# Attention and feed-forward in one kernel: feed-forward work per step as a constant, or as a fixed step length less the step's attention work

## The reference

```python
scores = scale * np.matmul(q, k.transpose(0, 1, 3, 2))
kth = np.partition(scores, -32, axis=-1)[..., -32:-31]
scores = np.where(scores >= kth, scores, -1e9)
attn = softmax(scores)                      # with 1e-9 added to the sum
x = (attn @ v) as (2304, 512)
h = x @ w_in;   x = np.maximum(0.01 * h, h) @ w_out      # layer 0, 512 -> 2048 -> 512
h = x @ w_in2;  g = where(h >= 1, h, where(h <= -1, 0, (h + 1) ** 2 / 4))
out = g @ w_out2                                         # layer 1
```

## Time and profile before

| | |
|---|---|
| median of 3 runs | 1160.88 us (1160.45 to 1161.57) |
| the profiled execution | 1158.78 us |
| its span, first to last instruction | 1156.8 us |
| TensorE (PE) busy | 1092.0 us, 94% |
| VectorE (DVE) busy | 872.2 us, 75% |
| ScalarE (ACT) busy | 792.0 us, 68% |
| GpSimd (POOL) busy | 472.1 us, 41% |
| chain that ended last, by engine | PE 79%, DVE 8%, ACT 6%, POOL 2%, issue 2%, DMA 2% |

### The profile page before, as it was taken

How to read it: one execution, slowest core, us unless ns; L and a number is a source line. 1 busy time by engine, 2 the same in 40 slices (tenths; PEclk the granted TensorE clock), 3 DMA queues, 4 the chain that set the end, 5 groups by cost and what they waited for, 6 DMA issues and landing times.

```text
span 1156.8 us, 21227 instructions
## 1 busy us (share of the span) xinstructions
PE 1092.0 (94%) x7568; PEld 1003.4 (87%) x7568; DVE 872.2 (75%) x1914; ACT 792.0 (68%) x1827; POOL 472.1 (41%) x500
## 2 busy tenths in 40 slices
PE   5557998899999999999999999999999999999998
PEld 3336888799989999999998879998899999999998
DVE  7999978889899998999979979988994005300234
ACT  7887989877798777887779758678786224322332
POOL 5645559652363332642236324134441234222322
PEclk9969999999999999999999989999999999999999
DMA  7998998788667788788666656656456677787774
GB/s 246 348 344 297 378 323 293 272 307 302 217 218 256 246 309 294 284 293 289 236 227 243 242 186 241 209 194 208 151 193 227 202 253 255 254 292 254 254 248 135
DMA packets 90680, 295.51 MB, mean 255 GB/s; under 512 B 10065, under 2 KB 13777, under 8 KB 90577
## 3 DMA queue, kind: packets, MB, share of 16 engines
q1 hardware_dynamic: 86544, 289.45, 71.2%
q10 hardware_dynamic: 4032, 4.72, 1.1%
HBM read 255.85 MB, written 38.27 MB: 254 GB/s over the span
## 4 chain that ended last, share of the span: by engine, by line
PE 79%; DVE 8%; ACT 6%; POOL 2%; issue 2%; DMA 2%; SPq 0%; POOLq 0%; ACTq 0%; DVEq 0%
PE ps_f L936 21%; PE ps_f L944 20%; PE ps_f L937 20%; PE ps_av L895 7%; DVE top L1223 4%; DVE work L1227 3%; PE ps_s L856 3%; PE ps_t L872 2%; PE ps_t L878 2%; PE ps_t L856 1%; DMA raw<-wd 1%; DVE part_r L1250 1%; ACT probs L1064 1%; POOL gate L747 1%; ACT scores L1035 1%
## 5 line engine op out<-in xcount | busy, mean ns | idle before, releaser
L1223 DVE MAX8 top<-work 128x8 f32<-128x576 f32 x432 | 310.6, 744 | 0.2
L936 PE MATMUL ps_f<-xy,w_ring 128*128 128x384 f32 (+2 forms) x896 | 288.8, 322 | 4.0 <-ACT part_o L1119 2.0
L936 PE MATMUL ps_f<-gate,w_ring 128*128 128x384 f32 (+2 forms) x896 | 286.7, 320 | 0.0
L944 PE MATMUL ps_f<-gate,w_ring 128*128 128x384 f32 (+2 forms) x896 | 281.7, 314 | 3.4 <-POOL gate L747 3.3
L944 PE MATMUL ps_f<-xy,w_ring 128*128 128x384 f32 (+2 forms) x896 | 280.8, 313 | 1.3 <-POOL xy L757 0.6
L937 PE MATMUL ps_f<-gate,w_ring 128*128 128x384 f32 (+2 forms) x896 | 281.0, 314 | 0.0
L937 PE MATMUL ps_f<-xy,w_ring 128*128 128x384 f32 (+2 forms) x896 | 280.2, 313 | 0.0
L1227 DVE MATCH_REPLACE8 work<-top,work 128x576 f32<-128x576 f32 x288 | 213.5, 741 | 0.0
L747 POOL TENSOR_TENSOR gate<-part_r,gate 128x384 fp32r<-128x384 f32 (+2 forms) x112 | 101.4, 906 | 240.0 <-ACT gate L1123 239.5
L936 PEld LDWEIGHTS ps_f<-xy,w_ring 128*128 128x128 f32 x896 | 169.2, 189 | 17.1 <-issue 9.6
L1258 DVE TENSOR_TENSOR y_acc<-ps_f,y_acc 128x384 f32<-128x384 f32 (+2 forms) x56 | 27.7, 495 | 199.1 <-PE ps_f L944 199.0
(11 more groups left out here) (85 smaller groups left out, 1846.2 us busy)
## 6 DMA issues: line engine op xcount, KB each, us to landing
w_ring<-w_split SPq DMA_DIRECT2D x408, 512.0 KB, 4.2
w_split<-w_ring SPq DMA_DIRECT2D x40, 512.0 KB, 6.1
raw<-wd SPq DMA_DIRECT2D x64, 256.0 KB, 5.4
w_split<-xy SPq DMA_DIRECT2D x24, 512.0 KB, 4.8
v_sb<-vd SPq DMA_DIRECT2D x32, 320.0 KB, 5.9
kq<-kqd SPq DMA_DIRECT2D x16, 480.0 KB, 3.7
kq<-kqd SPq DMA_DIRECT2D x15, 416.0 KB, 5.7
out_t<-y_acc ACTq DMA_DIRECT2D x12, 192.0 KB, 4.1
```

Of the source, the lines that this page charges most:

```text
L936: pe.matmul(out, w[:, 0, m], high, start=first, stop=False)
L944: mm = pe.matmul(out, w[:, 0, m], low, start=False, stop=end)
L1223: op = dve.max(top[:, t % TOP_SLOTS, 8 * r:8 * r + 8], source(t, r))
```

## The change

The constant FILL is taken out. Each of the steps 41 to 151 now adds STEP_NS less `attention_ns(s)`, a sum of fixed prices for the scores, the transposition and the values that the step holds. Earlier steps add FIRST_FILL as before. Nothing else of the program is edited; what else differs follows from the plan.

```diff
-FILL = 4275.0
+STEP_NS = 5950.0
...
+def attention_ns(s):
+
+    scores = sum(score_step(it) == s for it in ITEMS)
+    moved = [2 * KC + 1 if not it.mixed else KC + 2 for it in ITEMS if out_step(it) == s]
+    widths = [GROUP_WIDTH[gp // PAIRS % 2] for gp in range(GROUPS) if values_step(gp) == s]
+    return 1160.0 * scores + sum(109.0 * n + 100.0 for n in moved) + sum(20 * w / 2.4 + 300.0 for w in widths)
...
-        credit += FILL if s >= READY[1] else FIRST_FILL
+        credit += STEP_NS - attention_ns(s) if s >= READY[1] else FIRST_FILL
```

## The result

| | before | after |
|---|---|---|
| median | 1160.68 us (4 runs beside those of after) | 1169.53 us (4 runs, 1168.70 to 1170.11) |
| ratio to before | | 1.0078 [1.0062, 1.0094] |
| profiled execution, span | 1158.78, 1156.8 us | 1169.38, 1167.6 us |
| steps 41 to 151 | 677.42 us | 680.90 us |
| the tail | 253.45 us | 259.85 us |

The change makes the kernel 0.8% slower: 8.9 us, where 4.4 us less were forecast. The first view is the page of the kernel after, its busy time and its chain by engine.

A forecast was written before the change was run, and what follows sets the result against it. TensorE was taken to bound the kernel. Its losses in steps 41 to 151 were to fall from 13.7 to 5.9 + 2.0 + 1.0 + 0.4 = 9.3 us, so 1160.88 - 4.4 = 1156.5 us, range 1152.5 to 1162.5.

The forecast's parts named there:

- What bounds the kernel, and the views: TensorE bounds steps 41 to 151 and the tail; the change can only move time lost between its items.
- Point 1: Steps 41 to 151: TensorE's step lengths become more even, standard deviation 1.22 us instead of 1.64.
- Point 2: Three hidden units, 6.24 us, leave steps 41 to 151 and enter the tail: net 0.
- Point 3: Five places where score and transposition follow each other with little or no cover: 5.9 us lost together.
- Point 4: Output unit 3b1o0 opens in step 115 and waits for gates: 2.0 us lost instead of 2.87, clock kept.
- Point 5: Other late copies and gates, laid to VectorE lags over 33 us, mostly go: 1.0 us kept, bounds 0 and 5.
- Point 6: Weight loads on SP's queue, and POOL's and ScalarE's operations at other places: no cost, 0 us.
- Rival A: Late gate copies in ScalarE's order hold ps_t copies at three of five new adjacencies: slower, 1165.5 us, chance 0.12.
- Rival C: Gates and copies never late, only the five adjacencies remain: 7.4 us less, 1153.5 us, chance 0.12.
- B: Rival: waits only move, 3b1o0's opening at step 115 costs as much as now: 1160.9 us, chance 0.28.

The follow-up runs named there:

- e5: Third and fourth MAX8 of every VectorE tile read half the columns: kernel before 1151.48 us, kernel after 1156.06 us.
- g4: Four gate buffers instead of three, three v buffers instead of four: kernel before 1158.62 us, kernel after 1166.7 us.
- e10: Kernel after with third and fourth MAX8 of every VectorE tile on half the columns and four gate buffers: 1154.74 us.
- e2: Kernel before with FILL 4218 instead of 4275, so three more units stand in the tail, no attention price: 1162.22 us.
- e8: Kernel before with the price's sign turned, so steps with more attention get more units, same number in all: 1170.13 us.
- e4: Kernel after with STEP_NS 6007 instead of 5950, as many units ahead of the tail as in before: 1161.79 us.
- e7: Kernel after with STEP_NS 6030 instead of 5950, five more units in steps 41 to 151: 1171.30 us.
- e13: Kernel before with output unit 3b1o1 moved from step 115 to 114, between score 63 and transposition 59: 1157.58 us.
- e14: e13 with four gate buffers and three of v: 1156.95 us.
- e11: Kernel before with step 114's score ahead of unit 3b1o0, four gate buffers and three of v: 1160.28 us.
- e12: e8 with the third and fourth MAX8 of every VectorE tile on half the columns: 1158.56 us.

## Why the prediction was wrong, point by point

**What bounds the kernel, and the views**: right. TensorE's work is the same and all of the difference lies between its items.

**Point 1, length of steps**: right as far as it goes (the steps are more even and the longest lag is shorter, though 32.8 us where 31 was worked out). What was concluded from it was not.

**Point 2, three units into the tail**: right, 6.24 us forecast, 6.40 measured.

**Point 3, pairs**: right in place, a little short in size: 5.9 forecast, 6.9 measured. Each place: 1.0, 1.0, 1.6, 1.5 and 0.8 against 1.02 (step 78), 1.53 (124), 1.62 (130), 1.83 (140) and 0.91 (105). Of these 124 is furthest off: its nearest row, 1.17 us, was taken down to 1.0 for the half clock in it.

**Point 4, opening of 3b1o0**: right, 2.0 forecast, 1.7 measured, and the clock stayed at 1.00. The opening of 4b0o0 in step 139 adds 1.1 that the text had put among the copies that go (137's 0.90).

**Point 5, copies and gates late elsewhere**: this step failed. It took the late copies of before for the work of a large lag, over 33 us, and kept 1.0 us for the rest. Measured: 12.0 us of late copies with no lag over 32.8, and this is more than the upper bound of 5 that the text gave. The row it rested on (step 105, 33.5 us) shows that a large lag can go with a late copy, not that a small one excludes it. And four of the five losses that it let go had no such lag in before: only step 136 stands over 33 us (33.4), while step 57 is at 29.9, step 82 at 29.3, step 110 at 31.0 and step 137 at 28.5. For step 57 it is the distance from TensorE's first product of the step to VectorE's tile 59, both in the kernel before:

```profile
320.57 0.39 PE L936 MATMUL ps_f<-xy,w_ring 128*128 128x320 f32 x1
```

```profile
350.46 0.75 DVE L1223 MAX8 top<-scores 128x8 f32<-128x576 f32 x1
```

What the runs showed in its place: a copy is late where the plan leaves too little between the item that ScalarE has to copy and the next one that needs it, given what stands ahead of that copy in ScalarE's order. Of that, 7 us here go with the chain of gates over VectorE and POOL (e5, g4, e10). Of the 5 us that stay, 1.9 are ScalarE's own order (487.18: the same in e10, and shortened with the exponential ahead of the copy); 0.9, at the transposition of step 82, still have a wait for POOL behind them; the rest was not taken apart. In the plan of before these meetings are rare: it has the fewest late copies of the eight plans tried (5.3 against 9.0 to 14.2). Whoever reads the trace of before sees a kernel in which they don't show and takes them for absent. The prediction treated the placing of 104 steps' units as neutral outside the five pairs; it is the largest term.

**Point 6, queues**: wrong by 2.1 us. That before shows no wait for weights in these steps doesn't show how much room there was. In steps 44 and 45 units of the new plan come before their weights have landed (249.01 and 254.68). These waits are absent in the flat plans (before, e2) and in e8, and there in all five plans whose price of attention has the change's sign, 1.0 to 2.1 us. Why those two loads are late, no run here tested.

**The rivals.** Rival A (slower, 1165.5 us, chance 0.12) had the sign and the mechanism, ScalarE in order behind late gate copies. It looked for it in the five pairs, at 14.9 us, where the loss was 6.9; the rest, 3.4 in its sum, was 18.1. Rival C's reason (lags of 31 us or less cause no large loss) is refuted by the same numbers as point 5. The range ended at 1162.5: it added the edge of B, not the edge of point 5, whose own upper bound of 5 us was too low because it came from the sum seen before and not from what one place can cost (2.3 us in the trace of before, up to 2.5 in e4 and e7) times the places that could be hit.

**What stays open.** Why before's plan has so few late copies: neither the standard deviation of its steps nor the level nor the mean lag orders them. Of the 5 us that stay with a lighter chain, ScalarE's order is shown at one place (1.9 us); the cause of the rest is not shown. That a late copy needs too little cover in the plan is read from the places that were followed, not tested at each. The clock ahead of step 41 (0.91 against 0.95, 0.9 us) has no cause in the plan and wasn't followed up.

## What to carry to other kernels

Where four engines run in fixed orders and hand results to each other within 1 to 3 us, the average length of a step says little: list every hand-over (who copies, what stands ahead of that copy in its engine's order, how much cover is between) for the new plan, and price each, before believing that an even plan is a faster one. A plan that a profile shows nearly free of such waits is a point from which most moves lose; price a reshuffle of all units as the mean over other plans (here 9 to 14 us of late copies), not by the waits of the one plan that was measured. And when one item in a step is the trouble, move that item (e13, e14) instead of changing the rule for all.

## What the runs showed that I had not expected

**The clock and the length of a wait.** The size of a wait alone doesn't say whether the half clock follows. In e13 two waits of 0.47 and 1.40 us with a few products between them (2.96 us of loss) are followed by products at the half clock, and e14 loses as much there and has the same granted clock. In after a loss of 1.7 us at the same opening is not, nor is a loss of 2.26 us at step 136 of before, nor one of 2.4 us ahead of the transposition of step 82 in e4, where 1.00 is granted from 475 to 505:

```profile
484.40 0.41 PE L880 MATMUL ps_t<-ident,probs 128*128 128x128 f32 x2 [2.16 <-issue]
```

But in e14 a wait of 1.66 us at step 136 is followed by a values product at the half clock, 3.94 us for sixteen matmuls, 1.7 us lost, with 0.94 granted from 795 to 825 (e11 and e12 have the same there, 0.94 in both):

```profile
807.02 0.37 PE L858 MATMUL ps_s<-kq_split 64*128 64x288 f32 x1 [1.66 <-ACT p_rem L1086]
...
808.00 3.94 PE L897 MATMUL ps_av<-p_t,v_sb 128*64 128x320 f32 x16
```

The kernel before with four gate buffers has the same wait at the same place, 1.66 us, and differs from e14 only in steps 114 and 115. Its values product runs at the full clock, 2.37 us for the same sixteen matmuls, with 1.00 granted from 795 to 825:

```profile
807.85 0.37 PE L856 MATMUL ps_s<-kq_split 64*128 64x288 f32 x1 [1.66 <-ACT p_rem L1084]
...
808.84 2.37 PE L895 MATMUL ps_av<-p_t,v_sb 128*64 128x320 f32 x16
```

The Trainium skill ("TensorE: Matmul & The Clock Gate", section "HAM oscillation") warns that idling can bring the half clock back and slow the work behind the gap. The traces agree in e14, and not at the same wait of the kernel before with four buffers; nothing read here tells the two cases apart. It also eats gains: in e14 the four buffers shorten the loss at step 136 by 0.3 us, and 1.7 are lost behind it.

**A lighter ScalarE hardly helps.** 37 us less work on an engine that the chain of waits names for 6% of the span took 0.6 us off the losses of the stage.
